# Attention in the first third of a slot, the same unit's gated steps behind it, and the border by halves of the columns

## What is computed

```python
# 1: gated linear attention, q, k, v, a of shape (4, 8, 768, 48)
mag = sqrt(a_re**2 + a_im**2); scale = minimum(mag, 0.999) / (mag + 1e-06)
for t in range(S):
    S_re, S_im = ar * S_re - ai * S_im + outer(k[t], v[t]), ar * S_im + ai * S_re
    y[t] = q[t] @ S_re
# 2: x = y as (3072, 384); gated layer, d_ff = 1536
x = ((x @ w_a) * (x @ w_b)) @ w_out
# 3: top-1 of 8 experts for rows with x @ w_skip > 0, f = 1024
out = x; out[do] += gate * (relu(x[do] @ w1[e]) @ w2[e])
```

## Time and profile before

| | |
|---|---|
| median of 3 runs | 1191.31 us (1190.95 to 1192.48) |
| the profiled execution | 1189.92 us |
| its span, first to last instruction | 1188.1 us |
| mean granted TensorE clock | 0.913 |
| busy: PE, DVE, ACT, POOL | 907.3, 818.9, 368.9, 248.9 us |
| VectorE idle before magnitude, by ScalarE's squares | 41.1 us, 16 times |
| ScalarE idle for the load of gre | 44.0 us, 7 times |

### The profile page before, as it was taken

The page is one execution under the profiler, slowest core; times in us unless marked ns, Lnnn a source line. Parts: engine busy times, 40 slices in busy tenths (PEclk is TensorE's granted clock), DMA queues, the critical chain, the costliest instruction groups (busy, mean ns, idle before and its releaser), DMA issues. The chain is left out here.

```text
span 1188.1 us, 15277 instructions
## 1 busy us (share of the span) xinstructions
PE 907.3 (76%) x5652; PEld 809.2 (68%) x5652; DVE 818.9 (69%) x1375; ACT 368.9 (31%) x650; POOL 248.9 (21%) x188
## 2 busy tenths in 40 slices
PE   0002335997988899888889989889999992199997
PEld 0001335876877788767778878787888881199997
DVE  4986998799599889939987996997110004266672
ACT  4013103513522441342136135213222211154551
POOL 0515103112211311221141123114111113501001
PEclk9999665999989999888999989899999995599999
DMA  8211304002300410230141023001011117457650
GB/s 239 63 36 44 126 0 113 27 22 72 107 28 21 133 55 21 67 108 20 28 133 47 21 72 109 27 21 47 28 28 47 34 33 278 155 200 238 206 193 22
DMA packets 47949, 97.15 MB, mean 82 GB/s; under 512 B 4774, under 2 KB 39096, under 8 KB 47872
## 3 DMA queue, kind: packets, MB, share of 16 engines
q1 hardware_dynamic: 31632, 72.91, 19.5%
q10 hardware_dynamic: 13680, 18.68, 5.7%
q0 software_dynamic: 2560, 4.51, 1.0%
HBM read 83.70 MB, written 15.77 MB: 84 GB/s over the span
## 5 line engine op out<-in xcount | busy, mean ns | idle before, releaser
L812 POOL TENSOR_TENSOR s_gsb<-s_asb,s_bsb 128x384 f32<-128x384 f32 x96 | 105.6, 1100 | 621.1 <-ACT s_bsb L481 621.1
L238 PE MATMUL ps<-s_wo,s_gsb 128*128 128x384 f32 x576 | 203.9, 490 | 4.8 <-issue 4.8
L260 PE MATMUL ps<-s_qk 48*128 48x128 f32 x384 | 49.3, 341 | 177.6 <-DVE s_qk L679 105.4
L260 PEld LDWEIGHTS ps<-s_qk 48*128 48x128 f32 x384 | 37.5, 236 | 182.1 <-issue 107.1
L238 PEld LDWEIGHTS ps<-s_wo,s_gsb 128*128 128x128 f32 x576 | 108.0, 191 | 56.5 <-issue 6.1
L227 PE MATMUL ps<-s_xh,s_wah 128*128 128x384 f32 x288 | 83.9, 403 | 21.6 <-ACT s_bsb L481 10.8
L479 ACT COPY s_asb<-ps 128x384 f32<-128x384 f32 x96 | 45.9, 478 | 95.9 <-PE ps L227 95.9
L227 PEld LDWEIGHTS ps<-s_xh,s_wah 128*128 128x128 f32 x288 | 51.9, 210 | 29.6 <-ACT s_bsb L481 14.0
L481 ACT COPY s_bsb<-ps 128x384 f32<-128x384 f32 x96 | 46.2, 481 | 78.4 <-PE ps L227 78.4
L227 PE MATMUL ps<-s_xl,s_wah 128*128 128x384 f32 x288 | 69.7, 352 | 0.0
L227 PE MATMUL ps<-s_xh,s_wal 128*128 128x384 f32 x288 | 67.3, 342 | 0.0
(11 more groups left out here) (181 smaller groups left out, 2140.9 us busy)
## 6 DMA issues: line engine op xcount, KB each, us to landing
s_wo<-in_w_out ACTq DMA_DIRECT2D x95, 192.0 KB, 2.4
e_w1s<-in_w SPq DMA_DIRECT2D x8, 1536.0 KB, 7.1
e_w2s<-in_w SPq DMA_DIRECT2D x8, 1536.0 KB, 7.3
s_gre<-in_are_t SPq DMA_DIRECT2D x8, 672.0 KB, 7.2
s_gim<-in_aim_t SPq DMA_DIRECT2D x8, 672.0 KB, 5.3
s_qk<-in_k_t SPq DMA_DIRECT2D x8, 672.0 KB, 7.6
s_qk<-in_q_t SPq DMA_DIRECT2D x8, 672.0 KB, 5.4
s_vt<-in_v_t SPq DMA_DIRECT2D x8, 576.0 KB, 6.8
```

The source lines that it names most:

```text
L238: mm = pe.matmul(ps[:, DOWN + t, 0:DM], gsb[:, n % 2, t * P:(t + 1) * P], wo[:, n % WO_BUFS], start=(n == 0), stop=(n == NF1 - 1))
L260: mm = pe.matmul(ps[:, SC + v, pr * CH:(pr + 1) * CH], lanes(kf, pr, j, v), lanes(qf, pr, j, v), start=(c == 0), stop=(c == 1))
L812: pool.tensor_tensor(gsb[:, x % 2], asb[:, x % 2], bsb[:, x % 2], ALU.mult).then_inc(s["g_ready"], 1)
```

## The change

Everything is recast into nine slots. In slot u all three chunks of the attention of unit u stand in the first third, among the last four gated steps (LEAD = 4) of unit u-1. Behind them come gated steps 0 to 7 of unit u itself, and the routing of unit u-1. An `up` is given by its two banks apart (`up(n, 0)`, `up(n, 1)`) and each waits only for its own bank's copy. ScalarE's part is in the same order, with root and inverse by halves between the attention's copies; squares2 and inverse2 stand behind the copies of step 10. VectorE adds the chunk's part to the state (`added`) apart from the rest of `state`; newton and scale are called by halves; low_part(2) comes before the products in blocks, and those, state(2), the spreads, norm and the factors come in one piece at the end. GpSimd's two `keys` stand behind all twelve products. At the border gre is loaded by halves, each when factors has read the old half (semaphore re_free), squares of a half wait for that half of q and k alone, and `scores(0)` takes the first two pairs of heads when the first half is there. On SP's queue the loads of keys and queries stand before the stores of rows. In slot 0 the gated steps wait for the split weights piece by piece.

```diff
             def load_real(u):
+                for i, x in enumerate(PARTS):
+                    if not isinstance(u, int) or u > 0:
+                        sp.wait_ge(s["re_free"], 2 * (u - 1) + i + 1)
+                    sp.dma_start(gre[:LANES, x], pick(are_t, u)[:, x]).then_inc(s["ld_re"][i], 16)
...
     def scores(j):
         if j == 0:
-            pe.wait_ge(s["q_made"], 4 * (u + 1))
-            pe.wait_ge(s["k_made"], 4 * (u + 1))
...
         for pr in range(PAIRS):
+            if j == 0 and pr % (PAIRS // 2) == 0:
+                pe.wait_ge(s["q_made"], 4 * u + pr // (PAIRS // 2) * 2 + 2)
+                pe.wait_ge(s["k_made"], 4 * u + pr // (PAIRS // 2) * 2 + 2)
...
# TensorE, one slot (has_att and has_last left out)
+    scores(0); turn_keys(0, 0); up(0, 0); turn_keys(0, 1); up(0, 1)
+    adds(0); values(0); down(-1); turn_values(0); up(1, 0)
+    scores(1); turn_keys(1, 0); up(1, 1); turn_keys(1, 1); down(0)
+    adds(1); values(1); up(2, 0); turn_values(1); up(2, 1)
+    scores(2); turn_keys(2, 0); down(1); turn_keys(2, 1); up(3, 0)
+    adds(2); values(2); up(3, 1); turn_values(2); down(2)
+    down(3)
+    for n in range(LEAD, NF1):
+        up(n, 0); up(n, 1)
+        if n > LEAD: down(n - 1)
+        t = n - LEAD - 1
+        if has_last and 1 <= t <= CU: route_logits(t - 1)
+        if has_last and 0 <= t < CU: route_turn(t)
# ScalarE, one slot
+    prep(squares); keys(0, 0); gate(0, 0); prep(root, 0); keys(0, 1); gate(0, 1)
+    values(0); prep(root, 1); high_part(0); gate(1, 0)
+    keys(1, 0); prep(inverse, 0); gate(1, 1); keys(1, 1); values(1); gate(2, 0)
+    high_part(1); prep(inverse, 1); gate(2, 1)
+    keys(2, 0); keys(2, 1); gate(3, 0); values(2); gate(3, 1); high_part(2)
+    rows_out()
+    for n in range(LEAD, NF1):
+        gate(n, 0); gate(n, 1)
+        t = n - LEAD - 1
+        if has_last and 1 <= t <= CU: logits(t - 1)
+        if has_last and 0 <= t < CU: turned(t)
+        if n == NF1 - 2: prep(squares2); prep(inverse2)
# VectorE, one slot
     magnitude(); masked(0)
-    newton(); scale(); state(0); first_products(); low_part(0); in_blocks()
-    masked(1); totals(); state(1); carry_spread(); low_part(1); last_spread()
-    masked(2); norm(); factors0(); factors1(); state(2); low_part(2)
+    newton(0); added(0); state(0); low_part(0)
+    newton(1); masked(1); scale(0); added(1); state(1); low_part(1)
+    scale(1); masked(2); scaled(); added(2); low_part(2)
+    blocks(); state(2); spreads(); last()
# GpSimd, one slot
     for n in range(NF1):
         product(...)
-        if has_prep and n >= NF1 - 2:
-            keys(u + 1, 1 - par, n - (NF1 - 2))
+    for i in range(2):
+        keys(u + 1, 1 - par, i)
```

More of the change, by code:

```diff
@@ L216, in at_least @@
                         pe.wait_ge(s[name], n)
[L218 to L229, removed]
@@ L335, in route_logits @@
                     mm.then_inc(s["lg_ready"], 1)
[L337 to L368, removed]
@@ new lines, in slot @@
+                if has_att:
+                    scores(0)
+                    turn_keys(0, 0)
+                up(0, 0)
+                if has_att:
+                    turn_keys(0, 1)
+                up(0, 1)
+                if has_att:
+                    adds(0)
+                    values(0)
+                down(-1)
+                if has_att:
+                    turn_values(0)
+                up(1, 0)
+                if has_att:
+                    scores(1)
+                    turn_keys(1, 0)
@@ new lines, in slot @@
+                up(1, 1)
+                if has_att:
+                    turn_keys(1, 1)
+                down(0)
+                if has_att:
+                    adds(1)
+                    values(1)
+                up(2, 0)
+                if has_att:
+                    turn_values(1)
+                up(2, 1)
+                if has_att:
+                    scores(2)
+                    turn_keys(2, 0)
+                down(1)
+                if has_att:
+                    turn_keys(2, 1)
@@ L428, in inverse2 @@
                     act.activation(gim[L, par, 0, x], gim[L, par, 0, x], ACT.Exp, scale=-1.0).then_inc(s["nr0"], 1)
-            prep = (squares, root, inverse, squares2, inverse2)
-            PREP_AT = ((0, "first"), (0, "behind"), (1, "behind"), (8, "before"), (8, "behind"))
             def slot(b, par):
@@ new lines, in prep @@
+                def prep(part, *half):
+                    if has_prep:
+                        part(u + 1, 1 - par, *half)
+                prep(squares)
+                if has_att:
+                    keys(0, 0)
+                gate(0, 0)
+                prep(root, 0)
+                if has_att:
+                    keys(0, 1)
+                gate(0, 1)
+                if has_att:
+                    values(0)
+                prep(root, 1)
+                if has_att:
+                    high_part(0)
@@ new lines, in slot @@
+                gate(1, 0)
+                if has_att:
+                    keys(1, 0)
+                prep(inverse, 0)
+                gate(1, 1)
+                if has_att:
+                    keys(1, 1)
+                    values(1)
+                gate(2, 0)
+                if has_att:
+                    high_part(1)
+                prep(inverse, 1)
+                gate(2, 1)
+                if has_att:
+                    keys(2, 0)
+                    keys(2, 1)
+                gate(3, 0)
@@ L519, in _ @@
             act.wait_ge(s["ld_const"], 16)
-            for part in prep:
-                part(0, 0)
-            slots_of(slot, NU + 1)(act)
+            squares(0, 0)
+            for i in range(2):
+                root(0, 0, i)
+            for i in range(2):
+                inverse(0, 0, i)
+            squares2(0, 0)
+            inverse2(0, 0)
+            slots_of(slot, NU)(act)
         @block.vector
@@ L705, in slot @@
                     base[0] = 0
-                parts = preparation(u + 1, 1 - par) if not static or u < NU - 1 else (lambda: None,) * 11
+                nothing = lambda *half: None
+                parts = preparation(u + 1, 1 - par) if not static or u < NU - 1 else (nothing,) * 7
                 def at_least(name, n):
@@ L788, in _ @@
             link(dve.memset(ylast[:], 0.0))
-            for part in preparation(0, 0):
-                part()
+            magnitude, newton, scale, scaled, blocks, spreads, last = preparation(0, 0)
+            magnitude()
+            for i in range(2):
+                newton(i)
+            for i in range(2):
+                scale(i)
+            scaled()
+            blocks()
+            spreads()
+            last()
             dve.wait_ge(s["ld_const"], 16)
```

333 lines of the change are left out of this document (177 added, 156 removed).

## The result

| | before | after |
|---|---|---|
| median of runs | 1191.2 us | 1216.1 us (4 runs, 1212.6 to 1216.8) |
| ratio | | 1.0201, 95% interval 1.0188 to 1.0214 |
| profiled span | 1188.1 | 1214.9 |
| mean granted clock | 0.913 | 0.910 |

The change makes the kernel 2% slower. The forecast was 1185 us, half a per cent down, with a range to 1207: wrong in sign and in range.

The account below looks back on a forecast made before the run. VectorE's preparation and TensorE, both near full, were taken to bound six units, TensorE alone the tail. From 1189.9 us, -47.0 + 24.6 + 17.2, less about 1, gave 1183.7; with the median 1.4 above, 1185 us, range 1161 to 1207.

Parts of the forecast that it names:

- The tail: TensorE's work after VectorE's last factors, to the last down: 113.3 us in place of 160.3, 47.0 us saved.
- F: End of low_part(2), counted from the end of the previous factors: forecast 48.5 us in odd units, 46.7 in even.
- The answer of ScalarE before the factors: VectorE's wait between spreads and factors, expected wholly exposed in the new order: 4.8 us.
- The load by halves: Border load of gre, issued behind the factors' first products: taken as hidden; without that cover up to 8 us a unit.
- The loop jump: TensorE's jump at mid-loop, expected to fall into border idle time: 0 to 5 us gained, about 1 taken off.
- Part 4: Run from low_part(2) to the factors' end; with the first third, a unit of 107.3 against 103.2, six times, +24.6 us.
- E7: Instant VectorE finishes unit 7's factors, handing q and k to TensorE; forecast to move later than 820.
- The factors: VectorE's last piece of each unit, with GpSimd's keys beside it: 16.4 us, between bounds 14.9 and 16.4.
- Part 5: First unit, attention standing alone on the chain mostly at half clock: 113 us in place of 95.8, +17.2.
- (a): Faster rival: full clock in slot 0 and later units 2.5 us tighter each, 1157 us; chance 0.24.
- (b): Slower rival: in chunk 0 TensorE's wait for keys(0,1) drops its clock; 3 us a unit, +18, 1203 us; chance 0.22.
- (c): Slower rival: late gated steps delay ScalarE's squares2, VectorE waits 2 us a unit; +13, 1198 us; 0.14 with another rival.

Follow-up runs that it names:

- e3: Changed kernel with GpSimd's keys on 16 of 768 columns (rest of k unscaled, output not the reference's): 1172.5 us.
- e7: Changed kernel with the four ups of the first third cut to a third of their products (output not the reference's): 1197.7 us.
- e5: Changed kernel with the old border: gre in one load behind the last factor, squares and scores(0) waiting for all of q and k: 1240.6 us.
- e2: Kernel before the change with GpSimd's gated product on 16 of 384 columns, the rest left out: 1157.8 us.
- e1: Changed kernel with GpSimd's gated product on 16 of 384 columns (output not the reference's): 1177.6 us.
- e6: Changed kernel with the first block product moved ahead of low_part(2): 1192.1 us, ratio to the kernel before 1.0005.
- e9: Changed kernel with ScalarE's order alone altered: root and inverse ahead of the attention's copies, squares2 one step earlier; 1202.9 us.
- e11: Kernel e8 with a second block product moved ahead of low_part(2): 1153.6 us, ratio 0.9662.
- e8: Changed kernel with e9's ScalarE order and VectorE's first third reordered, first block product and low parts earlier, state(2) behind spreads: 1167.8 us, ratio 0.9805.
- e4: Kernel before the change with only the border by halves (gre load, squares, scores(0)): 1188.5 us, ratio 0.9990.

## Why the prediction was wrong

**Right, part by part.** The tail: 113.3 us forecast, 113.4 measured. The first third: F at 46.7 and 48.5 forecast, 46.4 to 48.9 measured, with 1.0 to 1.6 us where TensorE was to wait 1.8 for the keys. In the first unit 53 was forecast and 53.9 measured, in part by luck: in e3 and e7, with the same work in that third, it came at 57.3. VectorE's idle time in the third, some 15 us forecast, is 48.0 - 32.8 = 15.2. The answer of ScalarE before the factors: 4.8 and 4.8. The load by halves: hidden, 3.4 us a half (median of 16); e5 prices the whole border at 3.0 us a unit. The load's first half was issued 16 us before E, the second 7, as the factors' first products allow. The loop jump: no unit of the changed kernel stands out, where one of before took 108.8.

**Wrong: Part 4, the run from F to the next E.** It was put at 61.4 us (even) and 58.6 (odd) and took 65.0 and 62.4: 3.7 too little, six times, and 5.0 in the first unit. With smaller rests, E7 came at 891.9 in place of 862.1; this is all of the miss but 3 us (2.0 in the experts, 1 that I had taken off for the loop jump). Two terms of the sum were mis-sized.

- The stretch from block products to spreads was taken over from the earlier trace rows, less the pieces that leave it: 40.2 and 37.4. It took 43.0 and 40.5. The row held five gated products of GpSimd beside it, for 2.5 us (e2); in the new order seven lie there, at 0.73 each, 5.1 us (e1). This is 2.6 of the 2.8 and 3.1 us that were missing; where the rest lies is open. I had counted the products on TensorE's and ScalarE's side and costed their effect on VectorE at nothing, though the earlier trace rows had shown what GpSimd does to VectorE and I had used it for the keys.
- The factors, 16.4, were priced without product(11), which now runs beside factors(0): 17.2, and 16.4 again without the products (e1).

The forecast also took off 0.3 us a unit because the row at 443 was "a little long"; in the mean of the six units the stretch of before takes 43.6 us against its 43.7, so that only 0.1 was due.

Part 5 took over the same run, with the same error: in the kernel before, no product lay beside the stretch of that unit, and seven came to it. The bounds for the factors, 14.9 to 16.4, were missed above.

**The sign.** Before the measurement the sum was -47.0 for the tail against +24.6 and +17.2. The measured terms are -46.9, +48.5 and +23.0. The first term needed the other two to stay below 47; the point from which the period decides, 108.3 at the forecast first unit, stood inside what a fault of 1 us in the run would reach. The range ended 22 us above the forecast, 3.1 us for each of the seven units; the run from F to E alone took 3.7 more in six of them and 5.0 in the first.

**The rivals.** (a) did not come. (b) did not come in the changed kernel, whose wait stayed at 1.0 to 1.6 us, but in e7 the clock fell behind a wait of 1.95. (c) did not come: the answer before the factors stayed at 4.8. In odd units it grew to 6 in e6, where VectorE was 4 us earlier, and to 7 in e1, so the margin was as thin as said.

**Why the layout loses, then.** A unit costs 8.1 us more: 3.6 of VectorE's work and 4.5 of its waiting. VectorE has 87 us of work before and 91 after. Both layouts lose 8 us of it to GpSimd's products, so these are not what parts them. The change adds 2.4 in the factors (keys of both halves beside them) and takes the slack: all of VectorE's waiting is gathered in the first third, where TensorE's and ScalarE's chain cannot be shortened by any of it (e9), while behind F nothing but the factors' answer is waited for and each microsecond is paid (e3, and e1 in even units). What was missing is work for VectorE in the third: with 7 us of block products moved there and ScalarE out of the way the same layout is 3.4% faster than the kernel before (e11).

Open: e8 against e9 and e6 does not part what low_part ahead of state, the earlier scale(1) and state(2) behind the spreads are worth one by one; and what an early load of gre is worth in the old order (e4) is measured at two borders only.

## What to carry to other kernels

When work is moved from a place where its engine waits to one where the engine is the chain, its duration has to be taken anew: count, from the other engine's rows, how many of its operations will lie beside it, and give each a price. A gap before an instruction names its last releaser, not the chain: before closing it, ask what the next steps wait for (e9, and e4 at E1). A load that is freed early is early only if nothing ahead of it on its queue waits: read the time of its issue before judging the edit (e4). And a layout is not judged before the free time that it makes has been given work.

## What the runs showed of the hardware that I had not expected

A GpSimd operation costs VectorE a large share of its own length. Twelve 128x384 products of about 1.1 us each take 8 us out of VectorE (e1, e2), 0.73 each in its unbroken run, and a 112x768 operation of VectorE goes from 1.02 to 2.60 us beside keys of 1.80 and 2.40. But VectorE's mask and low part, which read one of their inputs from PSUM (the ps of their rows), are not longer beside a product: eight masks in the kernel before and seven low parts in the changed one, each overlapping a product by about 0.5 us, took at most 0.02 us more than the shortest. The Trainium skill, "SBUF — State Buffer", section "SBUF: two separate sides", says of the shared pair of ports that the one which starts first gets it for the whole instruction and the other fully blocks; 1.6 us of delay beside an operation of 1.8 agrees with that.

A TensorE that needs less can run slower: with 8 us of products fewer in the first third (e7), its clock fell back to 1.2 GHz in four of six units, behind waits of 1.95 to 2.54 us, where the changed kernel's waits of 1.0 to 1.6 had left it at full.
